# Attention inside a fused mixer: the second head's token halves on swapped partitions, score-value products in one lot

## The chip, the cores and the metric

The kernel runs on one core of one Trainium2 chip. The metric is the device time of one execution in microseconds (us). Before the change the median of three runs is 686.84 us (686.51 to 688.32).

## The reference, cut to what matters

```
# q, k, v, alpha: batch 4, heads 8, seq 768, head_dim 48
for t in range(S):
    state = alpha[:, :, t, :, None] * state + einsum('bhd,bhe->bhde', k[:, :, t], v[:, :, t])
    y[:, :, t] = einsum('bhd,bhde->bhe', q[:, :, t], state)
x = y with its heads side by side                      # 768 tokens x 384
u = x + (V^T U^T over the tokens) applied to x         # low rank, 32
x = u + relu(u @ w_ch1) @ w_ch2                        # hidden width 1536
theta = x @ w_theta;  y = w_tok_r (x cos theta) + w_tok_i (x sin theta)
u = x + y;  out = u + relu(u @ w_ch)
```

Everything is fp32. The large products are made from three products of split operands each (high x high, high x low, low x high).

## The kernel before, in words

**Units.** The attention of one batch element is worked off in eight units (`UNITS`): four pairs of heads, each in two halves of 384 tokens. A unit has three chunks (`c`) of 128 tokens, and each chunk has two sub-chunks of 64 tokens (`p` = 0, 1). The two heads of a pair are `h` = 0, 1. TensorE's array is used as four quarters of 64 x 64. A product's input partitions (0 to 63 or 64 to 127) choose the row of the quarter, its output partitions the column. All products of the attention are small, and each has two records in the profile, so a lot of 12 products shows as x24.

**The four steps of a unit on TensorE.**

- `pe_scores` (line 401): for each `h`, `p`, `c` it multiplies decayed keys (`k_end`) with an identity and the scaled queries (`ident_q`). This gives at once the keys turned round, so that tokens lie on partitions, and the scores. Input row `h`, output column `p`: all four quarters. Twelve products.
- `pe_state` (line 442): keys (`k_nat`) times values (`v_sb`), the contribution of each sub-chunk to the state. Input row `p`, output column `h`: all four quarters. Twelve products. It begins with a wait (below).
- the carried part of the output (line 491): scaled queries times the state before the sub-chunk. Row `h`, column `p`: four quarters. Twelve products for odd units; ten for even ones, whose first sub-chunk has no state before it.
- the score-value products (lines 497 and 507): masked scores (`probs`) times values. Row `p`, column `p`: only two of the quarters. Twelve products in two lots of six: line 497 in `pe_output_first`, line 507 in `pe_output_second`.

**Between them.** ScalarE copies the keys out of PSUM (`k_nat`, line 415), the state's contributions (`updates`, 463), the output (`x_nat`, 576). VectorE masks the scores (`probs`, 426) and runs three scans per unit (`tail` 342, `rel` 354, `state` 470). GpSimd makes `k_end` (379) and `ident_q` (370). SP issues all loads. `load_v` waits for `y_ready` of eight units earlier, and `queries` for an earlier `y_ready` as well.

**The first batch element** has nothing to hide behind. `pe_scores(u+1)`, some filling (two full-array products of `keep_warm`, line 1429, or part of the low-rank product, lines 589 and 643), `pe_output_first(u)` after `st_done`, `pe_state(u+1)`, a wait of TensorE for its own `half_done`, and `pe_output_second(u)` follow each other.

**The later three** are woven into the MLP of the element before. That MLP goes through 24 slots of 18 full-array products (lines 695 and 725). Every second slot ends with `pe_group(k)`, for `k` = 0 to 8, and group 9 comes in a slot near the end. Group `k` does the output of unit `k-2`, the scores of unit `k` and the state of unit `k-1`, as far as these exist. All operands are waited for ahead of the group (`group_ready`), so within a group TensorE waits only for its own earlier products. Those waits keep two row quarters from writing the same PSUM bank and partitions at once. Before the change they are: `half_done` (after line 497, ahead of `pe_state`) and `scores_ready` (ahead of line 507). Groups 2 to 7 have both, groups 8 and 9 only the first, groups 0 and 1 none.

**PSUM.** Later elements have banks 0, 1 and 2 for all of it. Scores of the two heads are in banks 0 and 2, the state's contributions of `p` = 0 and 1 in banks 0 and 1, the output of the two heads in banks 1 and 2. In every lot of the kernel before, products of row 0 and products of row 1 write different banks.

Of the kernel before, what the change touches and what calls it, by code (L numbers as in the profile page):

```python
# [61 lines left out]
def mixer_kernel(nc, qka, v_nat, u_w, v_w, w1, w2, w_theta, tok_r, tok_i, w_ch, out_t, x2_dram):  # L62
    ctx = ExitStack()
    with ctx:
# [210 lines left out]
        def y_ps(b, u):  # L275
            i, j = y_banks(b)
            return banks[:, i:j + 1, SCORES:SCORES + OUT].rearrange("p h (c n) -> p c h n", c=CPH)

        def updates_ps(b, u):
            (i, at), (j, to) = update_places(b, u)  # L280
            step = 512 * (j - i) + to - at
            two = banks[0:PAIR_ROWS, i:i + 2, :].rearrange("p i x -> p (i x)")
            if first_batch(b):
                two = two.rearrange("p (s x) -> p s x", s=2)[:, :, at:at + OUT]
            else:
                two = two[:, at:at + 2 * step].rearrange("p (s x) -> p s x", s=2)[:, :, 0:OUT]
            return two.rearrange("p s (c n) -> p n c s", c=CPH)
# [30 lines left out]
        def side(p):  # L318
            return slice(SUB * p, SUB * (p + 1))

# [69 lines left out]
        def pe_scores(pe, b, u):  # L390
            n, s = UNITS * b + u, u % 2
            i, j = score_banks(b, u)
            if first_batch(b):
                pe.wait_ge(S["k_end_done"], n + 1)
                pe.wait_ge(S["q_rel_done"], n + 1)
                wait(pe, S["updates_done"], updates_before(b, u - 1) if u else 0)
            for c in range(CPH):
                for p in range(2):
                    for h, ps in ((0, bank[i]), (1, bank[j])):
                        g = 2 * c + p  # L400
                        last = nc.tensor.matmul(ps[side(p), Q_STEP * c:Q_STEP * (c + 1)], k_end[s][rows(h), sub(g)],  # L401
                                                q_slot(u)[rows(h), g, :], stop=True, skip_group_check=True,
                                                start=first_batch(b) or c == 0 and (h == 0 or u < 2))
            return last
# [24 lines left out]

        def pe_state(pe, b, u):  # L430
            n, s = UNITS * b + u, u % 2
            if first_batch(b):
                pe.wait_ge(S["k_nat_done"], n + 1)
                pe.wait_ge(S["mask_done"], n + 1)
                pe.wait_ge(S[f"v_in{u}"], 16)
            for c in range(CPH):
                for p, (i, at) in enumerate(update_places(b, u)):
                    cols = slice(at + HEAD_DIM * c, at + HEAD_DIM * (c + 1))
                    for h in range(2):
                        at = HEAD_DIM * (CPH * h + c)  # L440
                        wide = HEAD_ROW if h == 0 else HEAD_DIM
                        last = nc.tensor.matmul(bank[i][HEAD_ROW * h:HEAD_ROW * h + wide, cols],  # L442
                                                k_nat[s][side(p), :, :, :].rearrange("p h c n -> p (h c n)")[:, at:at + wide],
                                                v_sb[u][side(p), c, HEAD_DIM * h:HEAD_DIM * (h + 1)],
                                                stop=True, skip_group_check=True,
                                                start=first_batch(b) or c == 0 and u == (0 if p else UNITS - 1))
            last.then_inc(S["ds_ready"], 1)
# [30 lines left out]
        def pe_output_first(pe, b, u):  # L478
            n, s = UNITS * b + u, u % 2
            y0, y1 = (bank[i] for i in y_banks(b))  # L480
            if first_batch(b):
                pe.wait_ge(S["st_done"], n + 1)
                wait(pe, S["y_done"], n)
            for c in range(CPH):
                for p in range(2):
                    g = 2 * c + p
                    if g == 0 and u % 2 == 0:
                        continue
                    begins = c == (1 if u % 2 == 0 and p == 0 else 0)
                    for h, ps in ((0, y0), (1, y1)):  # L490
                        nc.tensor.matmul(y_tile(ps, p, c), q_slot(u)[rows(h), g, HEAD_DIM:], state[s][rows(h), :, g + 1],  # L491
                                         start=begins, stop=False, skip_group_check=True)
            if first_batch(b):
                pe.wait_ge(S["mask_done"], n + 1)
            for c in range(CPH):
                for h, p, ps in ((0, 0, y0), (1, 1, y1)):
                    last = nc.tensor.matmul(y_tile(ps, p, c), probs[s][side(p), h, c, :],  # L497
                                            v_sb[u][side(p), c, HEAD_DIM * h:HEAD_DIM * (h + 1)],
                                            start=False, stop=True, skip_group_check=True)
            return last  # L500

        def pe_output_second(pe, b, u):
            s = u % 2
            y0, y1 = (bank[i] for i in y_banks(b))
            for c in range(CPH):
                for h, p, ps in ((0, 1, y0), (1, 0, y1)):
                    last = nc.tensor.matmul(y_tile(ps, p, c), probs[s][side(p), h, c, :],  # L507
                                            v_sb[u][side(p), c, HEAD_DIM * h:HEAD_DIM * (h + 1)],
                                            start=False, stop=True, skip_group_check=True)
# [28 lines left out]
        def pe_group(pe, b, k):  # L538
            n = UNITS * b + k
            if k > 1:  # L540
                pe_output_first(pe, b, k - 2).then_inc(S["half_done"], 1)
            if k < UNITS:
                pe_scores(pe, b, k).then_inc(S["scores_ready"], 1)
            if k > 1:
                pe.wait_ge(S["half_done"], n - 1)
            if 0 < k <= UNITS:
                pe_state(pe, b, k - 1)
            if 1 < k < UNITS:
                pe.wait_ge(S["scores_ready"], n + 1)
            if k > 1:  # L550
                pe_output_second(pe, b, k - 2)
# [880 lines left out]
        def _(pe):  # L1432
# [9 lines left out]
            for u in range(UNITS - 1):  # L1442
# [24 lines left out]
            pe_output_first(pe, 0, UNITS - 1).then_inc(S["half_done"], 1)  # L1467
            pe.wait_ge(S["x_t_done"], 1)
            lr_turn(pe, 0, 0, 2).then_inc(S["first_turned"], 1)
            pe.wait_ge(S["half_done"], UNITS)  # L1470
            pe_output_second(pe, 0, UNITS - 1)
# [57 lines left out]
```

## Time and profile before

| | |
|---|---|
| median of 3 runs | 686.84 us |
| profiled execution, own time | 687.91 us |
| its span from first to last instruction | 686.2 us |
| granted TensorE clock, mean | 0.993 |
| TensorE busy | 666.6 us (97%) |
| VectorE, ScalarE, GpSimd busy | 338.1, 246.5, 250.6 us |
| records of the attention's products | L401 768, L442 768, L491 704, L497 384, L507 384 |

"Busy" of TensorE counts overlapping products once, and it does not say whether one, two or four quarters work. For small products one has to look at the distance between the starts in the timeline.

### The profile page before, as it was taken

How to read it: one execution, taken by the hardware profiler on the slowest of the kernel's cores; microseconds unless marked ns; L12 is line 12 of the kernel's file. 1: busy time of each engine (PE TensorE's matmuls, PEld its weight loads, DVE VectorE, ACT ScalarE, POOL GpSimd, SP SyncE). 2: the span in 40 equal slices, each digit the busy share in tenths (PEclk: the TensorE clock that was granted, in tenths of full speed). 3: DMA queues.
4: the chain of work that ended last, by engine and by line, in shares of the span. 5: the costliest groups of instructions: out<-in, count | busy, mean ns of one | idle time of the engine just before them, and what ended most of it. 6: DMA issues, size and time to landing. Idle time of an engine off the chain costs nothing.

```text
span 686.2 us, 15688 instructions
## 1 busy us (share of the span) xinstructions
PE 666.6 (97%) x6360; PEld 639.2 (93%) x6360; DVE 338.1 (49%) x540; ACT 246.5 (36%) x519; POOL 250.6 (37%) x253
## 2 busy tenths in 40 slices
PE   7798999999999999999999999999999999999998
PEld 4477889999999999999999999999999999999998
DVE  7677786226555327555324124475545552554522
ACT  4464543323333223443223343435322431432220
POOL 5564763112333112333111364156332631643121
PEclk9899999999999999999999999999999999999999
DMA  9935613004414005401000643040022005002201
GB/s 254 238 105 129 182 42 115 1 2 126 108 39 115 1 2 146 111 15 37 1 1 35 230 128 93 1 149 24 1 81 104 23 11 172 23 0 69 70 0 70
DMA packets 25353, 52.36 MB, mean 76 GB/s; under 512 B 2144, under 2 KB 18128, under 8 KB 25296
## 3 DMA queue, kind: packets, MB, share of 16 engines
q1 hardware_dynamic: 25296, 51.52, 25.2%
q8 instruction: 45, 0.74, 0.5%
q14 instruction: 12, 0.10, 0.0%
HBM read 42.08 MB, written 9.44 MB: 75 GB/s over the span
## 4 chain that ended last, share of the span: by engine, by line
PE 89%; DVE 5%; issue 4%; ACT 2%; DMA 1%; SPq 0%; DVEq 0%; ACTq 0%
PE banks L695 21%; PE banks L1060 21%; PE banks L725 19%; PE banks L1132 6%; PE banks L978 5%; PE banks L491 3%; PE banks L401 3%; PE banks L1035 2%; PE banks L442 2%; PE banks L507 2%; PE banks L497 1%; PE banks L1429 1%; PE banks L643 1%; DMA qka_sb<-qka 1%; DVE rel L354 1%
## 5 line engine op out<-in xcount | busy, mean ns | idle before, releaser
L709 DVE SCALAR_TENSOR_TENSOR hidL<-banks,hidH 128x384 fp32r<-128x384 f32 x96 | 53.3, 555 | 119.9 <-ACT hidH L705 119.7
L695 PE MATMUL banks<-uH,w1H 128*128 128x384 f32 x288 | 100.0, 347 | 0.3 <-ACT uH L675 0.3
L725 PE MATMUL banks<-hidH,w2H 128*128 128x384 f32 x288 | 96.6, 335 | 1.3 <-ACT x_nat L576 0.7
L695 PE MATMUL banks<-uL,w1H 128*128 128x384 f32 x288 | 96.6, 335 | 0.0
L725 PE MATMUL banks<-hidH,w2L 128*128 128x384 f32 x288 | 96.5, 335 | 0.0
L695 PE MATMUL banks<-uH,w1L 128*128 128x384 f32 x288 | 96.5, 335 | 0.0
L725 PE MATMUL banks<-hidL,w2H 128*128 128x384 f32 x288 | 96.2, 334 | 0.0
L705 ACT ACTIVATE hidH<-banks 128x384 fp32r<-128x384 f32 x96 | 47.0, 490 | 117.9 <-PE banks L695 117.9
L379 POOL TENSOR_TENSOR k_end<-qka_sb,tail 112x384 f32<-112x384 f32 x32 | 30.0, 937 | 82.6 <-DVE tail L342 80.6
L1118 POOL TENSOR_TENSOR u2L<-x_res,u2H 128x384 fp32r<-128x384 f32 x24 | 24.4, 1017 | 95.5 <-ACT u2H L1112 95.5
L725 PEld LDWEIGHTS banks<-hidH,w2H 128*128 128x128 f32 x288 | 54.1, 188 | 2.7 <-issue 1.6
L695 PEld LDWEIGHTS banks<-uH,w1H 128*128 128x128 f32 x288 | 54.1, 188 | 2.5 <-issue 0.6
L695 PEld LDWEIGHTS banks<-uL,w1H 128*128 128x128 f32 x288 | 54.1, 188 | 0.3 <-DVE uL L680 0.3
L695 PEld LDWEIGHTS banks<-uH,w1L 128*128 128x128 f32 x288 | 54.1, 188 | 0.0
L725 PEld LDWEIGHTS banks<-hidL,w2H 128*128 128x128 f32 x288 | 54.1, 188 | 0.0
L725 PEld LDWEIGHTS banks<-hidH,w2L 128*128 128x128 f32 x288 | 54.1, 188 | 0.0
L354 DVE TENSOR_TENSOR_SCAN rel<-qka_sb,rel_start 112x390 f32<-112x390 f32 x32 | 52.9, 1653 | 1.4 <-DVE rel_start L350 0.3
L1060 PE MATMUL banks<-tokiH,ziH 128*128 128x384 f32 x144 | 49.4, 343 | 0.8 <-DVE tokiL L247 0.8
L1060 PE MATMUL banks<-tokrH,zrH 128*128 128x384 f32 x144 | 49.2, 342 | 0.0
L1060 PE MATMUL banks<-tokrH,zrL 128*128 128x384 f32 x144 | 48.4, 336 | 0.0
L1060 PE MATMUL banks<-tokrL,zrH 128*128 128x384 f32 x144 | 48.4, 336 | 0.0
L370 POOL TENSOR_TENSOR ident_q<-qka_sb,rel 112x384 f32<-112x384 f32 x31 | 30.1, 971 | 49.9 <-PE banks L507 26.7
(133 smaller groups left out, 1446.5 us busy)
## 6 DMA issues: line engine op xcount, KB each, us to landing
qka_sb<-qka SPq DMA_DIRECT2D x31, 507.1 KB, 6.4
v_sb<-v_nat SPq DMA_DIRECT2D x32, 144.0 KB, 6.5
stage<-w SPq DMA_DIRECT2D x6, 768.0 KB, 9.1
x_dram<-u_t SPq DMA_DIRECT2D x8, 576.0 KB, 3.7
x_f<-x_dram SPq DMA_DIRECT2D x12, 384.0 KB, 4.3
x_res<-x_dram SPq DMA_DIRECT2D x8, 576.0 KB, 4.3
out_t<-stage SPq DMA_DIRECT2D x24, 192.0 KB, 1.9
stage<-tok_r_t SPq DMA_DIRECT2D x3, 768.0 KB, 4.5
```

Source lines behind the costliest of these rows:

```text
L354: nc.vector.tensor_tensor_scan(flat(rel[0:PAIR_ROWS]), alpha_of(u)[:, 0:SCAN], rel_start[0:PAIR_ROWS, :], 0.0, ALU.mult, ALU.add).then_inc ...
L370: ops.tensor_tensor(q_slot(u)[0:PAIR_ROWS, :, HEAD_DIM:], q_of(u), rel[0:PAIR_ROWS, :, 1:SLOT], ALU.mult).then_inc(S["q_rel_done"], 1)
L379: nc.gpsimd.tensor_tensor(subs_of(k_end[s][0:PAIR_ROWS, :]), k_of(u), tail[s][0:PAIR_ROWS, :, 1:SLOT], ALU.mult).then_inc(S["k_end_done"], 1)
L401: last = nc.tensor.matmul(ps[side(p), Q_STEP * c:Q_STEP * (c + 1)], k_end[s][rows(h), sub(g)], q_slot(u)[rows(h), g, :], stop=True, skip_g ...
L695: last = nc.tensor.matmul(ps[:, 0:HALF], w[:, f, P * k:P * (k + 1)], x[half][:, k, :], start=(k == 0 and i == 0), stop=(k == DM_TILES - 1 ...
L705: nc.scalar.activation(hidH[s % 2][:], hid_ps[s % 2][:, 0:HALF], ACT.Relu).then_inc(S["hidH_done"], 1)
L709: nc.vector.scalar_tensor_tensor(hidL[s % 2][:], hid_ps[s % 2][:, 0:HALF], 0.0, hidH[s % 2][:].bitcast(F32), ALU.max, ALU.subtract).then_i ...
L725: last = nc.tensor.matmul(acc[m][:, 0:HALF], w[:, f, P * m:P * (m + 1)], x[s % 2][:], start=(f == 0 and i == 0), stop=(f == F_TILES - 1 an ...
L978: last = nc.tensor.matmul(th_ps[half][:, 0:HALF], w[:, k, P * m:P * (m + 1)], x[:, k, HALF * half:HALF * (half + 1)], start=(i == 0), stop ...
L1060: last = nc.tensor.matmul(tok_ps[half][:, 0:HALF], z[m][:, c, :], w[:, c, HALF * half:HALF * (half + 1)], start=(start and c == cs[0] and ...
L1118: nc.gpsimd.tensor_tensor(u2L[:, m, t], x_res[:, m, t], u2H[:, m, t].bitcast(F32), ALU.subtract).then_inc(S["u2L_done"], 1)
L1132: last = nc.tensor.matmul(ch_ps[t % 2][:, 0:HALF], w[:, k, P * m:P * (m + 1)], x[:, k, HALF * half:HALF * (half + 1)], start=(i == 0), sto ...
```

## The change

The second head of a pair keeps its two sub-chunks on swapped partitions. For `h` = 1 the scores, turned keys and values of sub-chunk `p` lie on the partitions of `1 - p` (`held(h, p)` = `side(p ^ h)`). The host lays `v_nat` out to match, at the same size. The score-value products then have input row `p ^ h` and output column `p`, and the state's contributions have input row `p ^ h` and output column `h`. The output and the state end where they did.

The score-value products become one lot of twelve (`pe_values`), which opens the output. The carried part (`pe_carried`) follows and ends it. A group's order is now: score-value products (unit `k-2`), state (unit `k-1`), carried part (unit `k-2`), scores (unit `k`). TensorE's waits for itself are `half_done` inside `pe_carried`, ahead of the first product with `(h, p)` = (1, 1), and `ds_ready` ahead of the scores. `half_done` is now given by one of the last four products of the state (by the last score-value product in group 9 and in the first element). Group 1 gets a wait it did not have. The banks of the later elements change places: scores in 1 and 2, output in 0 and 2, contributions in 0 and 1.

In the first element `pe_values` waits only for the mask and the output copy of the unit before. The wait for `st_done` stands in `pe_carried`.

```diff
         def score_banks(b, u):
-            return (i, i + 1) if first_batch(b) else (0, 2)
+            return (i, i + 1) if first_batch(b) else (1, 2)
         def update_places(b, u):
-            return ((i, SCORES), (i + 1, SCORES)) if first_batch(b) else ((0, SCORES), (1, 0))
+            return ((i, SCORES), (i + 1, SCORES)) if first_batch(b) else ((0, 0), (1, SCORES))
         def y_banks(b):
-            return (4, 5) if first_batch(b) else (1, 2)
+            return (4, 5) if first_batch(b) else (0, 2)
...
+        def held(h, p):
+            return side(p ^ h)
...
+        FOUR = ((1, 0), (0, 0), (1, 1), (0, 1))
+
         def pe_state(pe, b, u):
...
             for c in range(CPH):
-                for p, (i, at) in enumerate(update_places(b, u)):
+                for h, p in FOUR:
...
+                                            k_nat[s][held(h, p), :, :, :].rearrange("p h c n -> p (h c n)")[:, at:at + wide],
+                                            v_sb[u][held(h, p), c, HEAD_DIM * h:HEAD_DIM * (h + 1)],
...
+                    if not first_batch(b) and u and c == CPH - 1 and (h, p) == (1, 0):
+                        last.then_inc(S["half_done"], 1)
             last.then_inc(S["ds_ready"], 1)
...
+        def pe_values(pe, b, u):
+            n, s = UNITS * b + u, u % 2
+            if first_batch(b):
+                pe.wait_ge(S["mask_done"], n + 1)
+                wait(pe, S["y_done"], n)
+            for c in range(CPH):
+                for h, p in FOUR:
+                    last = nc.tensor.matmul(y_tile(bank[y_banks(b)[h]], p, c), probs[s][held(h, p), h, c, :],
+                                            v_sb[u][held(h, p), c, HEAD_DIM * h:HEAD_DIM * (h + 1)],
+                                            start=(c == 0), stop=False, skip_group_check=True)
+            return last
+
+        def pe_carried(pe, b, u):
+            n, s = UNITS * b + u, u % 2
+            if first_batch(b):
+                pe.wait_ge(S["st_done"], n + 1)
+            for c in range(CPH):
+                for h, p in FOUR:
+                    g = 2 * c + p
+                    if c == 0 and (h, p) == (1, 1):
+                        pe.wait_ge(S["half_done"], n + 1)
+                    if g == 0 and u % 2 == 0:
+                        continue
+                    last = nc.tensor.matmul(y_tile(bank[y_banks(b)[h]], p, c), q_slot(u)[rows(h), g, HEAD_DIM:],
+                                            state[s][rows(h), :, g + 1], start=False, stop=True,
+                                            skip_group_check=True)
             last.then_inc(S["y_ready"], 1)
...
         def pe_group(pe, b, k):
             n = UNITS * b + k
             if k > 1:
-                pe_output_first(pe, b, k - 2).then_inc(S["half_done"], 1)
-            if k < UNITS:
-                pe_scores(pe, b, k).then_inc(S["scores_ready"], 1)
-            if k > 1:
-                pe.wait_ge(S["half_done"], n - 1)
+                last = pe_values(pe, b, k - 2)
+                if k > UNITS:
+                    last.then_inc(S["half_done"], 1)
             if 0 < k <= UNITS:
                 pe_state(pe, b, k - 1)
-            if 1 < k < UNITS:
-                pe.wait_ge(S["scores_ready"], n + 1)
             if k > 1:
-                pe_output_second(pe, b, k - 2)
+                pe_carried(pe, b, k - 2)
+            if k < UNITS:
+                if k > 0:
+                    pe.wait_ge(S["ds_ready"], n)
+                pe_scores(pe, b, k).then_inc(S["scores_ready"], 1)
...
-                pe_output_first(pe, 0, u).then_inc(S["half_done"], 1)
+                pe_values(pe, 0, u).then_inc(S["half_done"], 1)
+                pe_carried(pe, 0, u)
                 pe_state(pe, 0, u + 1)
-                pe.wait_ge(S["half_done"], u + 1)
-                pe_output_second(pe, 0, u)
```

## Rows read from the trace of the kernel before

**Rows 1.** The page, its first line and the busy time of TensorE

```profile
span 686.2 us, 15688 instructions
PE 666.6 (97%) x6360; PEld 639.2 (93%) x6360; DVE 338.1 (49%) x540; ACT 246.5 (36%) x519; POOL 250.6 (37%) x253
```

**Rows 2.** Windows: length, busy of PE, PEld, DVE, ACT, POOL, clock, DMA, GB/s

```profile
0.00:54.00 54.00, 42.94 (x818) 31.12 (x819) 37.17 (x48) 27.60 (x62) 30.37 (x43) 0.91 0.75 201
54.00:82.00 28.00, 25.16 (x220) 22.63 (x220) 21.85 (x24) 13.00 (x31) 16.32 (x18) 1.00 0.52 140
...
88.00:190.00 102.00, 101.65 (x1224) 97.55 (x1225) 54.12 (x79) 36.33 (x85) 33.26 (x35) 1.00 0.24 70
```

**Rows 3.** Chain that ended last, 54 to 92 us: start, length, what

```profile
82.75 2.09 DVE rel L354
```

**Rows 4.** Groups by form: the two lots of score-value products

```profile
L497 PE MATMUL banks<-v_sb,probs 64*64 64x48 f32 x384 | 19.8, 221 | 0.0
L507 PE MATMUL banks<-v_sb,probs 64*64 64x48 f32 x384 | 18.1, 220 | 3.3 <-issue 3.1
```

**Rows 5.** Timeline of PE, group 1 of the second MLP: start, length, what

```profile
176.09 0.81 PE L401 MATMUL banks<-ident_q,k_end 48*64 48x112 f32 x24
176.71 0.50 PE L442 MATMUL banks<-v_sb,k_nat 64*64 64x48 f32 x24
177.15 0.45 PE L695 MATMUL banks<-uH,w1H 128*128 128x384 f32 x1
```

**Rows 6.** Timeline of PE, group 3, output of an odd unit

```profile
210.67 0.75 PE L491 MATMUL banks<-state,ident_q 48*64 48x48 f32 x24
211.23 0.46 PE L497 MATMUL banks<-v_sb,probs 64*64 64x48 f32 x9
...
212.10 0.56 PE L442 MATMUL banks<-v_sb,k_nat 64*48 64x48 f32 x23
212.47 0.55 PE L507 MATMUL banks<-v_sb,probs 64*64 64x48 f32 x12
212.95 0.44 PE L695 MATMUL banks<-uH,w1H 128*128 128x384 f32 x1
```

**Rows 7.** Timeline of PE, group 2, output of an even unit

```profile
202.02 0.65 PE L491 MATMUL banks<-state,ident_q 48*64 48x48 f32 x18
...
204.23 0.44 PE L695 MATMUL banks<-uH,w1H 128*128 128x384 f32 x1
```

**Rows 8.** Timeline of PE, group 8 (no scores)

```profile
236.83 0.65 PE L491 MATMUL banks<-state,ident_q 48*64 48x48 f32 x18
...
237.33 0.56 PE L497 MATMUL banks<-v_sb,probs 64*64 64x48 f32 x10
237.96 0.50 PE L442 MATMUL banks<-v_sb,k_nat 64*64 64x48 f32 x22
...
238.78 0.44 PE L695 MATMUL banks<-uH,w1H 128*128 128x384 f32 x1
```

**Rows 9.** Timeline of PE, group 9 (no scores, no state)

```profile
242.59 0.75 PE L491 MATMUL banks<-state,ident_q 48*64 48x48 f32 x24
243.14 0.54 PE L497 MATMUL banks<-v_sb,probs 64*64 64x48 f32 x12
243.73 0.55 PE L507 MATMUL banks<-v_sb,probs 64*64 64x48 f32 x12
244.22 0.44 PE L695 MATMUL banks<-uH,w1H 128*128 128x384 f32 x1
```

**Rows 10.** Chain that ended last, 0 to 60 us: a stall of TensorE

```profile
26.55 3.11 issue
```

**Rows 11.** Timeline of PE, last unit of the first element

```profile
50.21 0.75 PE L491 MATMUL banks<-state,ident_q 48*64 48x48 f32 x24 [0.39 <-DVE state L470]
50.77 0.53 PE L497 MATMUL banks<-v_sb,probs 64*64 64x48 f32 x12
...
51.70 0.55 PE L507 MATMUL banks<-v_sb,probs 64*64 64x48 f32 x12
```

More of the change, by code:

```diff
@@ L276, in y_ps @@
             i, j = y_banks(b)
-            return banks[:, i:j + 1, SCORES:SCORES + OUT].rearrange("p h (c n) -> p c h n", c=CPH)
+            return banks[:, i:j + 1:j - i, SCORES:SCORES + OUT].rearrange("p h (c n) -> p c h n", c=CPH)
         def updates_ps(b, u):
@@ L281, in updates_ps @@
             step = 512 * (j - i) + to - at
[L282 to L286, printed above, removed]
+            two = banks[0:PAIR_ROWS, i:i + 4, :].rearrange("p i x -> p (i x)")[:, 0:2 * step]
+            two = two.rearrange("p (s x) -> p s x", s=2)[:, :, at:at + OUT]
             return two.rearrange("p s (c n) -> p n c s", c=CPH)
@@ L400, in pe_scores @@
                         g = 2 * c + p
-                        last = nc.tensor.matmul(ps[side(p), Q_STEP * c:Q_STEP * (c + 1)], k_end[s][rows(h), sub(g)],
+                        last = nc.tensor.matmul(ps[held(h, p), Q_STEP * c:Q_STEP * (c + 1)], k_end[s][rows(h), sub(g)],
                                                 q_slot(u)[rows(h), g, :], stop=True, skip_group_check=True,
-                                                start=first_batch(b) or c == 0 and (h == 0 or u < 2))
+                                                start=first_batch(b) or c == 0 and u < 1 + h)
             return last
@@ L435, in pe_state @@
                 pe.wait_ge(S[f"v_in{u}"], 16)
+            places = update_places(b, u)
             for c in range(CPH):
-                for p, (i, at) in enumerate(update_places(b, u)):
+                for h, p in FOUR:
+                    i, at = places[p]
                     cols = slice(at + HEAD_DIM * c, at + HEAD_DIM * (c + 1))
[L439 to L446, printed above, removed]
+                    at = HEAD_DIM * (CPH * h + c)
+                    wide = HEAD_ROW if h == 0 else HEAD_DIM
+                    last = nc.tensor.matmul(bank[i][HEAD_ROW * h:HEAD_ROW * h + wide, cols],
+                                            k_nat[s][held(h, p), :, :, :].rearrange("p h c n -> p (h c n)")[:, at:at + wide],
+                                            v_sb[u][held(h, p), c, HEAD_DIM * h:HEAD_DIM * (h + 1)],
+                                            stop=True, skip_group_check=True,
+                                            start=first_batch(b) or c == 0 and (p == 1 or u == 0))
+                    if not first_batch(b) and u and c == CPH - 1 and (h, p) == (1, 0):
+                        last.then_inc(S["half_done"], 1)
             last.then_inc(S["ds_ready"], 1)
@@ L481, in pe_output_first @@
+        def pe_carried(pe, b, u):
+            n, s = UNITS * b + u, u % 2
             if first_batch(b):
                 pe.wait_ge(S["st_done"], n + 1)
-                wait(pe, S["y_done"], n)
             for c in range(CPH):
-                for p in range(2):
+                for h, p in FOUR:
                     g = 2 * c + p
+                    if c == 0 and (h, p) == (1, 1):
+                        pe.wait_ge(S["half_done"], n + 1)
                     if g == 0 and u % 2 == 0:
                         continue
[L489 to L509, printed above, removed]
+                    last = nc.tensor.matmul(y_tile(bank[y_banks(b)[h]], p, c), q_slot(u)[rows(h), g, HEAD_DIM:],
+                                            state[s][rows(h), :, g + 1], start=False, stop=True,
+                                            skip_group_check=True)
```

10 lines of the change are left out of this document (4 added, 6 removed).

## The prediction

> **What bounds the kernel now.** I read the page first: TensorE is busy for 666.6 of 686.2 us [rows 1]. Next I cut the span into stretches with their busy times [rows 2]. From 88 us on TensorE has hardly a gap (101.65 of 102.00 us), so every tenth of a microsecond taken from it there shortens the run. From 54 to 88 us it is different: TensorE has gaps, VectorE is busy for 21.85 of 28.00 us, and the chain of work runs through VectorE's scans until group 2 is past [rows 3]. Whatever TensorE gains or loses in groups 0, 1 and 2 of the first MLP is covered by them. Before 54 us TensorE, VectorE and the loads share the chain. Last I read the timeline of each kind of group. The three later elements repeat them to within 0.01 us, so one of each is shown [rows 5 to 9].
>
> **How a lot is priced.** A group costs from its first attention record to the next full-array record: 1.06 us for group 1 [rows 5], 2.28 for odd groups 3, 5, 7 [rows 6], 2.21 for even groups 2, 4, 6 [rows 7], 1.95 for group 8 [rows 8], 1.63 for group 9 [rows 9]. The pace of a lot is its length less the duration of one record, that is from first start to last start.
>
> - Six score-value products on two quarters (12 records) take 0.54 us with 0.22 for one record [rows 4, 9], a pace of 0.32. Twelve take 0.64 in two lots.
> - Twelve state products on four quarters (24 records of almost the same form) take 0.50 less 0.22 = 0.28 behind the scores [rows 5], and about 0.34 behind a wait or in a full group: 0.56 less 0.22 [rows 6], 0.50 less 0.22 for the first 22 of 24 [rows 8]. For twelve score-value products on four quarters I take 0.34, with 0.28 as the lower bound. The upper bound is the 0.64 of now.
> - The carried part has a pace of 0.48 (0.75 less 0.27), the scores 0.55 (0.81 less 0.26) [rows 5, 6].
> - A wait of TensorE for its own last product costs 0.28 from last start to next start: in group 9 the first lot ends at 243.68 and the next starts at 243.73, so 0.22 of record and 0.05 to 0.06 of waking [rows 9]. Without a wait a lot follows its predecessor in 0.02 to 0.07.
> - The full-array record behind a group starts 0.07 before the last small record ends: 242.59 to 244.22 against an end at 244.28 [rows 9].
>
> The Trainium skill ("TensorE: Matmul & The Clock Gate", section "Wait — 56ns, not 53.3ns?") says that starts never come closer than about 25 ns however small the product is. This trace disagrees: 24 starts in 0.28 us are 12 ns apart [rows 5]. By the page a lot of 24 would take an estimated 0.6 us, and four quarters would gain almost nothing; that is a rival below.
>
> **The change part by part.** The number of products, their shapes and all loads stay as they are. Work done by the host is no part of the time. ScalarE's copies read other banks with the same number of elements; I cost them at nothing, because ScalarE is busy for 36.33 of 102.00 us beside TensorE [rows 2], and if that cover were gone I would expect the same length of copy anyway.
>
> *Group 9.* Now: score-value 0.34, wait 0.28, carried 0.48, last record to full array 0.27 - 0.07 = 0.20. Sum 1.30 against 1.63: gain 0.33. (In an odd unit two carried products go ahead of the wait; that fills two quarters only, the other two still need their six records each, so I count nothing for it.)
>
> *Group 8.* Score-value 0.34, step 0.02, state 0.34, wait 0.26 (`half_done` comes from one of the last four state products, hardly earlier than the last one), carried 0.47, exit 0.20. Sum 1.63 against 1.95: gain 0.32. Before, this group had a bare wait too: the score-value lot ends at 237.89 and the state starts at 237.96 [rows 8].
>
> *Groups 2 to 7.* Before, both waits are hidden: other lots run between the product and the wait for it [rows 6]. Now the wait inside the carried part follows the state directly and is bare; the one for `ds_ready` ahead of the scores is hidden by the carried part. Score-value 0.34, step 0.02, state 0.34, wait 0.26, carried 0.47, step to the scores 0.08, scores 0.50 (no slow start behind a full-array product), exit 0.26 - 0.07 = 0.19. Sum 2.20 against 2.21 and 2.28: gain 0.01 in even and 0.07 in odd groups, 0.24 for the six. If the lots overlap better (state 0.28, wait 0.17) each gains 0.15 more; if each keeps a slow start, each loses 0.07.
>
> *Group 1.* State 0.34, a new bare wait 0.28, scores 0.55, exit 0.19. Sum 1.36 against 1.06: loss 0.30. Behind the waiting instruction stand only the scores, and ScalarE's and VectorE's work on them is due two slots later.
>
> *Three later elements.* 0.33 + 0.32 + 0.24 - 0.30 = 0.59 each, 1.8 in all. In the first MLP the loss of group 1 lies in the covered stretch: 0.3 back. So 2.1 us.
>
> *Order of the signals.* `scores_ready` still comes at the end of a group, where `y_ready` was; `y_ready` comes some 0.8 us earlier. ScalarE's first work after a group needs both, so it starts as before. `load_v` on SP and the queries on GpSimd wait for `y_ready` and can only go earlier. No queue is passed.
>
> *First element.* While TensorE is not waiting for `st_done` (units 0 to 4), the output costs 0.34 + 0.28 + 0.48 in place of 0.48 + 0.64 with its wait hidden: about even, at worst 0.1 us lost in each. Where it does wait for `st_done`, the score-value products now run ahead of that wait. In the last unit TensorE waits for VectorE's state [rows 11], and both lots behind it (0.32 each, with steps 0.8 in all) leave the chain, which from there runs through TensorE into the MLP. I take 0.8 - 0.3 = 0.5 us of gain, bounds -0.4 and +1.2. It passes through the covered stretch, since VectorE's chain there begins with the MLP.
>
> Sum: 2.1 + 0.5 = 2.6 us. The profiled execution's own time is 687.91 us (span 686.2), so it would be 685.3. The median of the runs is 1.07 us lower, 686.84, which gives **684.2 us**. With the bounds per group (+0.15 and -0.07, over nine groups in three elements +4 and -1.9, of which I believe half) this case alone spans 682.0 to 686.0.
>
> **The rivals.**
>
> - *The bare waits eat the gain (0.26).* The six middle groups are the weak term: 0.24 of gain rests on steps of 0.02 to 0.08. At 0.07 more in each of the 18, and nothing from the first element, 0.8 us are left: 686.0. For it: two hidden waits become one bare one, and group 1 gets a new one. Against it: groups 8 and 9 gain 0.3 each by rows alone.
> - *Two rows of quarters in one bank serialise (0.08), the case on the other side.* Before, products of row 0 and row 1 always write different banks within a lot. Now in the state and score-value lots both rows write into the same bank, in different partitions. No row shows that. If such products took turns, each lot of 24 would go at the two-quarter pace, 0.64 in place of 0.34: 0.3 us for eight state and eight score-value lots in each later element, 14.4 us, and some 2 us in the first, where only part of the lots lies on the chain: 686.84 - 2.6 + 16.4 = 700.6. It decides from 0.04 us a lot (2.6 us over 64 lots). The Trainium skill ("TensorEngine Tiling (Array Packing)", "Gotcha 1: PSUM Pressure") says that different row tiles cannot access the same PSUM bank at the same time, and does not say whether different partitions of it count. Nothing in this trace decides between them.
> - *A floor between starts (0.04).* If score-value products kept the pace of the scores (0.55) rather than the state's, 0.21 us for 24 units, 5.0 us, would be added: 689.2. Against it speaks the pace of the state [rows 5]. The 25 ns of the Trainium skill (the page and section above) would act in this way.
> - *Stalls of the first element move (0.10).* TensorE stands for 3.11 us in the middle of a lot, with no wait that a record names [rows 10], and its clock over the first 54 us is 0.91 [rows 2]. Such stalls may fall elsewhere with a new order of instructions, and a wait may then cover them or not: 3 us either way, 681.2 or 687.2, and in part with a lower clock behind them.
> - The likeliest case has 0.52.
>
> **How the numbers follow.** About 0.3%, 2.1 us, is what a measurement of this kernel can tell from no change. Of the likeliest case (centre 2.6 us of gain) most lies above it, but not all: 0.38 faster, 0.14 within. The waits' case: 0.05 faster, 0.17 within, 0.04 slower. Serialised and floor: slower, 0.12. Stalls: 0.06 faster, 0.02 within, 0.02 slower. Together faster 0.49, within 0.33, slower 0.18. The range is 681.4 to 687.6: it holds the first two cases and most of the stalls, and leaves out the 0.12 of the serialised cases.
>
> **What would show it.** In the profile after: groups 9 and 8 at 1.30 and 1.63, group 1 at 1.36, groups 2 to 7 all near 2.20 with no difference between odd and even; the score-value lot as x24 of some 0.56 us in length; a gap of 0.06 us between the state's end and the carried part. The state's pace tells of the bank: 0.34 as before, or 0.64. In the first element, full-array work should begin 0.5 us earlier than 53.5 us. The prediction is wrong if the six middle groups are off by more than 0.1 each, or if the first 54 us change by more than 1 us.

## The result, and the profile after

| | before | after |
|---|---|---|
| median | 688.32 us (5 runs, 686.51 to 689.11) | 682.64 us (5 runs, 681.54 to 684.83) |
| ratio | | 0.9938, 95% interval 0.9912 to 0.9964 |
| profiled execution, own time, span | 687.91, 686.2 | 684.83, 683.1 |

The change is faster by 0.6%, 4.3 us by the ratio and 5.7 by the medians. Two later sets with the same changed kernel gave 0.9917 (0.9896 to 0.9938) and 0.9931 (0.9906 to 0.9956). The kernel before had 56 runs in the three sets of experiments, with a median of 687.6 us. The changed kernel's medians were 682.14 and 683.46. So the gain is 4 to 6 us, where 2.6 was forecast; the interval of the first ratio alone reaches from 2.5 to 6.1 us. The profile of after is the slowest of its five runs, and it shows only 3.1 us of the gain.

The page of after, first line and busy times, against [rows 1]:

```profile
span 683.1 us, 15692 instructions
PE 663.4 (97%) x6360; PEld 631.3 (92%) x6360; DVE 337.3 (49%) x540; ACT 246.0 (36%) x519; POOL 250.3 (37%) x253
```

The timeline of TensorE in group 1 of the second MLP (start, length, what), against [rows 5], and below it the same group of the third:

```profile
175.05 0.56 PE L445 MATMUL banks<-v_sb,k_nat 64*48 64x48 f32 x24
175.69 0.81 PE L401 MATMUL banks<-ident_q,k_end 48*64 48x112 f32 x24
176.43 0.44 PE L694 MATMUL banks<-uH,w1H 128*128 128x384 f32 x1
...
275.61 0.56 PE L445 MATMUL banks<-v_sb,k_nat 64*48 64x48 f32 x24
```

The state ends at 175.61 and the scores begin at 175.69: this is the bare wait. The group takes 1.38 us where it took 1.06. From group 1 to group 1 of the next element it is 100.56 us. The kernel before starts the third MLP's group 1 at 277.66, 101.57 us after [rows 5]:

```profile
277.66 0.52 PE L401 MATMUL banks<-ident_q,k_end 48*64 48x112 f32 x12
```

So a later element is 1.01 us shorter. From the full-array product behind group 3 of the first MLP to the end of the span it is 592.2 us before and 589.0 after. The timeline of group 3 of after, against [rows 6]:

```profile
209.72 0.56 PE L490 MATMUL banks<-v_sb,probs 64*64 64x48 f32 x24
210.10 0.52 PE L445 MATMUL banks<-v_sb,k_nat 64*64 64x48 f32 x24
210.45 0.81 PE L506 MATMUL banks<-state,ident_q 48*64 48x48 f32 x22
...
211.12 0.81 PE L401 MATMUL banks<-ident_q,k_end 48*64 48x112 f32 x22
211.86 0.44 PE L694 MATMUL banks<-uH,w1H 128*128 128x384 f32 x1
```

The twelve score-value products are one lot of 24 records, 0.56 us long: a pace of 0.34 on four quarters. The state follows with 0.52 - 0.22 = 0.30, although rows 0 and 1 of the array now write into one bank. (In group 1, behind full-array products, it is 0.56 - 0.22 = 0.34.) The two carried products that are free of the wait start at 210.45. Group 2, 8 and 9 of after, the same view, against [rows 7], [rows 8] and [rows 9]:

```profile
201.12 0.57 PE L490 MATMUL banks<-v_sb,probs 64*64 64x48 f32 x24
201.51 0.52 PE L445 MATMUL banks<-v_sb,k_nat 64*64 64x48 f32 x24
202.01 0.66 PE L506 MATMUL banks<-state,ident_q 48*64 48x48 f32 x18
...
203.27 0.45 PE L694 MATMUL banks<-uH,w1H 128*128 128x384 f32 x1
...
235.47 0.56 PE L490 MATMUL banks<-v_sb,probs 64*64 64x48 f32 x24
...
237.03 0.45 PE L694 MATMUL banks<-uH,w1H 128*128 128x384 f32 x1
...
240.83 0.56 PE L490 MATMUL banks<-v_sb,probs 64*64 64x48 f32 x24
241.22 1.00 PE L506 MATMUL banks<-state,ident_q 48*64 48x48 f32 x24
242.15 0.44 PE L694 MATMUL banks<-uH,w1H 128*128 128x384 f32 x1
```

| group | before | forecast | after |
|---|---|---|---|
| 1 | 1.06 | 1.36 | 1.38 |
| 2, 4, 6 | 2.21 | 2.20 | 2.14 |
| 3, 5, 7 | 2.27 | 2.20 | 2.14 |
| 8 | 1.95 | 1.63 | 1.56 |
| 9 | 1.63 | 1.30 | 1.32 |

(Groups 3, 5 and 7 of before are 2.27 by the trace; the prediction's 2.28 is the difference of two rounded starts.) The gain is 0.21 in groups 2, 4 and 6, 0.40 in groups 3, 5 and 7, 0.39 in group 8 and 0.31 in group 9, less 0.32 in group 1: 1.0 us for each later element, in agreement with the period.

In the first element, the last unit's timeline, against [rows 11]:

```profile
49.90 0.56 PE L490 MATMUL banks<-v_sb,probs 64*64 64x48 f32 x24
50.57 0.76 PE L506 MATMUL banks<-state,ident_q 48*64 48x48 f32 x24
51.26 0.55 PE L642 MATMUL banks<-ident,x_nat 128*128 128x128 f32 x3
...
53.12 0.42 PE L694 MATMUL banks<-uH,w1H 128*128 128x384 f32 x1
```

The score-value lot lies ahead of the scan's end. From the carried part's start to the MLP's first product it is 2.55 us, where it was 53.5 - 50.21 = 3.3. The MLP begins only 0.4 us earlier than before, because the scan itself ends later (50.51 us against 50.16). Inside group 2 of the first MLP this execution has a stall, which the kernel before has not (chain of work, start, length, what):

```profile
83.10 1.35 issue
```

With it group 2 of the first MLP takes 3.89 us in place of 2.14.

### The profile page after: what moved, and what is told of

The parts are those of the page before. It is cut to its first block, busy times and chain, and to the rows that moved or that the text cites. A ratio compares the mean times of both kernels' runs of the same rounds, so it can differ in the third digit from the quotient of the medians.

```text
span 683.1 us, 15692 instructions
## 1 busy us (share of the span) xinstructions
PE 663.4 (97%) x6360; PEld 631.3 (92%) x6360; DVE 337.3 (49%) x540; ACT 246.0 (36%) x519; POOL 250.3 (37%) x253
## 4 chain that ended last, share of the span: by engine, by line
PE 93%; DVE 3%; issue 2%; ACT 1%; DMA 1%; SPq 0%; DVEq 0%; ACTq 0%
PE banks L694 23%; PE banks L724 21%; PE banks L1059 21%; PE banks L1131 6%; PE banks L977 5%; PE banks L506 3%; PE banks L401 3%; PE banks L1034 2%; PE banks L490 2%; PE banks L445 2%; PE banks L1428 1%; PE banks L642 1%; DMA qka_sb<-qka 1%; PE banks L588 1%; DVE tokiL L247 1%
## 5 line engine op out<-in xcount | busy, mean ns | idle before, releaser
L1059 PE MATMUL banks<-tokiL,ziH 128*128 128x384 f32 x144 | 48.3, 336 | 0.0
```

The source lines that it names most:

```text
L1059: last = nc.tensor.matmul(tok_ps[half][:, 0:HALF], z[m][:, c, :], w[:, c, HALF * half:HALF * (half + 1)], start=(start and c == cs[0] and ...
```

## The experiments

All times are medians. The kernel before is 687.85, 687.52 and 687.68 us in the three sets (e1 to e4, e5 to e8, e9 to e11).

### e1, e11: the changed kernel again

Edit: none.

> The changed kernel again, as the measure for the other three of this set. The theory (four quarters for the score-value lot, bare waits of TensorE for itself where hidden ones were) reads the changed kernel's groups from its own profile and expects them again to 0.01 us: 1.38 in group 1, 2.14 in groups 2 to 7, 1.56 in group 8, 1.32 in group 9, so 1.0 us gained in each later element. Whether the stall of 1.6 us between two starts inside group 2 of the first MLP, which the changed kernel's profile has and the kernel before has not, comes again is open: if it belongs to the new order it is there, if it is a matter of one execution it is not. Time expected 3 to 5 us under the kernel before.

> The changed kernel once more, beside these two. 4.5 to 6.5 us under the kernel before; no stall near 20 us; later elements as in its first profile to 0.02 us per group.

Measured: 682.14 us (6 runs, 679.75 to 684.41) and 683.46 us (8 runs, 680.73 to 685.66). e11 is 4.2 us under the kernel before, slightly less than expected. The groups repeat to 0.01 us, but for groups 2 and 3 of the first MLP. The stall in group 2 is absent from e1 and there again in e11, where the two groups take 3.07 and 2.50 us (chain of work, start, length, what):

```profile
81.82 0.53 issue
```

So it comes and goes with one and the same kernel. All profiles taken together, 7 of the 10 with the new order in the groups have it (after, e3, e4, e6, e7, e8, e11), e1, e2 and e10 have not, and none of the three with the old groups has it (the kernel before, e5, e9). The first product of the MLP comes at 50.59, 51.84 and, in the first profile, 53.12 us: the first element varies by 2.5 us with one kernel. From group 3 of the first MLP to the end the three profiles agree to 0.1 us.

### e2: the score-value lot head by head, on two quarters at a time

```diff
-            for c in range(CPH):
-                for h, p in FOUR:
+            for h in range(2):
+              for c in range(CPH):
+                for p in range(2):
                     last = nc.tensor.matmul(y_tile(bank[y_banks(b)[h]], p, c), probs[s][held(h, p), h, c, :],
```

> The same kernel, but the twelve score-value products are issued head by head: six of the first head on two quarters, then six of the second head on the other two. Products, waits and all other lots stay. Theory (the quarters are worth it): the lot takes the two-quarter pace, 0.64 in place of 0.35 us from first to last start, so each of groups 2 to 9 costs 0.2 to 0.3 more (the second half of the lot may run into the state's), 5 to 7 us over 24 units, and the whole change is lost: 1 to 3 us slower than the kernel before. Rival (the gain is in the order of the lots and one lot in place of two, not in the quarters): under 1 us of difference to the control.

Measured: 685.86 us, ratio to before 0.9972 (0.9955 to 0.9989), 3.7 us over the control. It was expected to be slower than the kernel before and is 2.0 us faster. Timeline of group 3 (start, length, what):

```profile
209.05 0.60 PE L491 MATMUL banks<-v_sb,probs 64*64 64x48 f32 x20
209.44 0.22 PE L445 MATMUL banks<-v_sb,k_nat 64*64 64x48 f32 x2
...
209.56 0.50 PE L445 MATMUL banks<-v_sb,k_nat 64*64 64x48 f32 x18
...
211.32 0.45 PE L695 MATMUL banks<-uH,w1H 128*128 128x384 f32 x1
```

The group takes 2.27 us, 0.13 more than with four quarters. The cost is half of what was expected, because the second head's six products run into the state's lot. With 0.12 to 0.13 for each of 24 groups that is 3.0 us: all that the later elements gain. From group 3 of the first MLP to the end it is 592.0 us, against 592.2 in the kernel before and 589.0 in the control. The quarters carry that gain, and the new order of lots alone gives nothing there. Yet the kernel stays 2 us under the one before. By this count the rest comes from the first element, which e9 tests.

### e3, e6: the old order in the first element alone

```diff
-                pe_values(pe, 0, u).then_inc(S["half_done"], 1)
-                pe_carried(pe, 0, u)
+                first_carried(pe, u)
                 pe_state(pe, 0, u + 1)
+                first_values(pe, u)
...
```

`first_carried` waits for `st_done` and gives `half_done`; `first_values` waits for `half_done` and gives `y_ready`. The last unit is changed in the same way.

> The changed kernel with the order of before in the first element alone: carried part after the state scan, the next unit's state, a wait for the carried part, then the twelve score-value products as one lot. The three later elements are untouched. Theory: in the last unit the score-value lot is back behind the scan and costs 0.4 to 0.6 us more from the scan's end to the MLP; units 0 to 4 are about even. So the first MLP product comes 0.3 to 0.6 us later than in the control and the time is 0.3 to 0.6 us longer. Rival (the order in the first element is worth nothing, loads and stalls decide there): the same start within 0.1 us.

> The kernel with the old order in the first element again, for a second profile. Theory: both stalls, the MLP begins between 53 and 56 us, against 50.5 to 53.1 us in the four profiles of the new order. Rival: no stall near 20 us, and a start within that band.

Measured: e3 685.46 us (7 runs, 683.26 to 689.18), ratio to before 0.9961 (0.9945 to 0.9978), 3.3 us over the control in the same set, where 0.3 to 0.6 was expected. e6, one execution: 686.76 us. The MLP begins at 56.05 in e3, whose profile is the slowest of its runs, and at 52.24 in e6; the latter lies under the expected band and inside that of the new order. Both profiles have a stall of TensorE near 20 us, 3.55 and 1.86 us long. Not all of the loss lies there: in both the stretch from the MLP's start through group 3 is longer too (table under e7).

### e5: the kernel before again

Edit: none.

> The kernel before, once more, for a second profile of its first 54 us. In its first profile TensorE stood twice with no wait that a record names: 1.7 us in the next unit's state products near 20 us and 3.1 us in the second score-value lot near 26 us. The profile of the kernel with the old order in the first element has both too (3.6 and 1.9 us); the four profiles with the new order have the second one alone. Theory (the early stall belongs to the old order): it is there again, 1.5 to 4 us long near 20 us, and the MLP begins between 52.5 and 56 us. Rival (chance): it is absent.

Measured: 685.98 us. The MLP begins at 51.58 us, 0.9 earlier than expected. The stall is there. It stands in TensorE's waits as "issue", in the middle of a lot of state products (timeline):

```profile
22.33 0.53 PE L442 MATMUL banks<-v_sb,k_nat 64*64 64x48 f32 x19 [1.82 <-issue]
```

### e7: only the wait moved, the new order of products kept

```diff
         def pe_values(pe, b, u):
             n, s = UNITS * b + u, u % 2
             if first_batch(b):
+                pe.wait_ge(S["st_done"], n + 1)
                 pe.wait_ge(S["mask_done"], n + 1)
```

> The changed kernel with the wait for the state scan moved ahead of the score-value lot in the first element; the order of the products is the new one. This splits the order from the wait. Theory A (the stall near 20 us comes when TensorE's instruction stream is held at the scan's wait ahead of the whole output, so that the next load of code is asked for late): the stall is back and the time is 2 to 3 us longer than the control's. Theory B (only the order of the products counts, or where the code is cut): no stall near 20 us; the time is 0.3 to 0.8 us longer, since the last unit's score-value lot (0.4) stands behind the scan again.

Measured: 685.88 us (12 runs), ratio to before 0.9980 (0.9957 to 1.0002). That is 3.7 and 2.4 us over the two controls, which ran in other sets, and 4.3 and 3.4 us by the ratios; 2 to 3 was expected. Of the two theories A is right as to the sign it named: the order of products is the new one, and the stall is back, at the same place in the stream of products (record 219 or 220 of TensorE's products in all five profiles that have it; timeline):

```profile
22.16 0.43 PE L507 MATMUL banks<-state,ident_q 48*64 48x48 f32 x9 [1.59 <-issue]
```

The DMA queues tell when the next piece of code was loaded. This is the view of the queues between 0 and 18.5 us, of e7 (its only line) and of the control e1:

```profile
q1 hardware_dynamic: 2041, 4.84, 92.6%
```

```profile
q1 hardware_dynamic: 2039, 4.82, 92.6%
q8 instruction: 1, 0.02, 0.3%
```

The loads in this time are the same to within two packets, and only the control has the instruction packet by then. All eight kernels with the score-value products ahead of the wait (the changed kernel and e1, e2, e4, e8, e9, e10, e11) have it before 18.5 us, and none of them stalls at this place of the stream. The five profiles with the wait ahead (the kernel before, e3, e5, e6, e7) have no such packet by 18.5 us and all stall there, for 1.6 to 3.6 us. The stall ends with the load: in these five traces the packet starts 2.6 to 3.0 us before the product at which TensorE stands. The same distance, 2.5 to 2.9 us, lies between the next packet and the end of the stall near 26 us, and between a later packet and the end of the stall in group 2 of the first MLP. Why the load is asked for later when TensorE is held ahead of the whole output is not shown by these runs.

That the wait's place costs time is shown by the medians. How much of it is the stall near 20 us is not. The profiles, cut at the MLP's first product and at the full-array product behind group 3 of the first MLP (us):

| | MLP begins | through group 3 | from there to the end |
|---|---|---|---|
| before, e5 | 53.49, 51.58 | 40.5, 40.5 | 592.2, 592.2 |
| e9 | 48.61 | 40.5 | 592.3 |
| after, e1, e11 | 53.12, 50.59, 51.84 | 41.0, 40.4, 40.7 | 589.0, 589.0, 588.9 |
| e3, e6 | 56.05, 52.24 | 42.2, 43.8 | 589.3, 589.0 |
| e7 | 51.83 | 42.3 | 589.1 |

e7 and the control e11 begin the MLP at the same time, although only e7 stood near 20 us. Of the 1.6 us between these two profiles 1.5 lie between the start of group 2 and the end of group 3 of the first MLP. There e7 has the stall of group 2 at twice the length, and behind it the granted clock is low, which it is not in e11 (chain of e7; windows of e7 and of e11 with length, busy of PE, PEld, DVE, ACT, POOL, clock, DMA, GB/s):

```profile
81.81 1.12 issue
```

```profile
83.00:86.40 3.40, 3.40 (x22) 3.25 (x22) 2.23 (x2) 0.96 (x4) 1.87 (x2) 0.64 0.02 6
```

```profile
82.40:86.00 3.60, 3.60 (x29) 3.42 (x29) 3.58 (x4) 2.06 (x6) 2.51 (x3) 1.00 0.01 5
```

e3 and e6 have such a low clock behind that stall as well (0.50 from 88 to 91 us, 0.59 from 85 to 89). In after, e11, e4 and e8, which have the stall too, the clock stays at 1.00 behind it. So what e3, e6 and e7 lose against the controls is in part a second loss, after the MLP's start. The kernel before does not have it, since its group 2 has no stall.

### e9: the new position in the first element, the old partitions

```diff
-                pe_output_first(pe, 0, u).then_inc(S["half_done"], 1)
+                first_values(pe, u)
+                first_carried(pe, u)
                 pe_state(pe, 0, u + 1)
-                pe.wait_ge(S["half_done"], u + 1)
-                pe_output_second(pe, 0, u)
...
```

`first_values` issues the twelve products on two quarters, ahead of the wait for the scan; `first_carried` waits for `st_done` and `half_done`. The last unit is changed in the same way.

> The kernel before, partitions and groups of the later elements as they were, but in the first element the twelve score-value products (on two quarters) go ahead of the wait for the state scan, and the carried part follows. Theory after the runs so far: about half of the change's gain is this position, not the swapped partitions, because TensorE no longer stands for 1.7 to 3.8 us near 20 us waiting for code. So the stall near 20 us is gone, the first packets of code beyond the preloaded ones come at 14 to 17 us rather than 19 to 22, and the time is 2.0 to 3.5 us under the kernel before. Rival: the stall's absence needs the new lot on four quarters or the other order of all lots; then the stall stays and the time is within 1 us of the kernel before.

Measured: 685.91 us (12 runs), ratio 0.9973 (0.9951 to 0.9994), 1.8 us under the kernel before (0.4 to 3.4 by the interval), a little less than expected. The stall near 20 us is gone, and the packet of code is there before 18.5 us. So the first element's part of the gain needs neither the swapped partitions nor four quarters. With the 3.0 us of the later elements it makes 4.8, against 4.2 to 5.7 of the controls. 1.8 us is also the length of the stall in the two profiles of the kernel before (1.67 and 1.82 us), but the gain is not that stall alone: the score-value products of the last unit leave the scan's path too, and a later wait can take up part of the stall. The chain of e9 shows what TensorE waits for next: the load of a unit's queries, keys and decays, then the scans (start, length, what):

```profile
7.24 11.76 DMA qka_sb<-qka
...
19.02 0.98 DVE tail L342
...
21.72 0.94 DVE state L470
```

### e4: the bare wait of groups 2 to 7 filled

```diff
...
+            score(b, k, 0, 1, 0)
+            for h, p, c in ((1, 0, first), (0, 0, first)):
+                carry(b, u, h, p, c)
+                todo.remove((h, p, c))
+            pe.wait_ge(S["vals_done"], (UNITS - 2) * (b - 1) + k - 1)
+            carry(b, u, 1, 1, 0)
+            todo.remove((1, 1, 0))
+            pe.wait_ge(S["half_done"], n - 1)
+            for x in todo:
+                last = carry(b, u, *x)
...
```

> The changed kernel with the bare wait of groups 2 to 7 filled: behind the state lot come one score product and up to three carried products that write no bank and partitions of the products waited for, one on each quarter; then the wait for half_done, the rest of the carried part and the rest of the scores. A second signal of TensorE to itself (after the score-value lot) covers the second head's carried product. Theory (the wait stands bare and costs its 0.2 us): groups 2 to 7 fall from 2.14 to 1.93 to 2.00 us, 18 of them, one of which lies under cover: 2.5 to 3.5 us under the control. Rival (a quarter is the bound, not the wait, or products are issued in order so that the fill pushes the rest back): groups stay at 2.10 or more and the time within 0.7 us of the control.

Measured: 680.10 us, ratio to before 0.9889 (0.9873 to 0.9906), 2.0 us under the control, where 2.5 to 3.5 was expected. Timeline of group 3 of the second MLP:

```profile
205.51 0.56 PE L522 MATMUL banks<-v_sb,probs 64*64 64x48 f32 x24
...
206.18 0.27 PE L408 MATMUL banks<-ident_q,k_end 48*64 48x112 f32 x1
206.19 0.26 PE L414 MATMUL banks<-state,ident_q 48*64 48x48 f32 x1
...
207.50 0.45 PE L731 MATMUL banks<-uH,w1H 128*128 128x384 f32 x1
```

The fill begins under the last state products (206.18), and the group takes 1.99 us in place of 2.14. Even groups take 1.96. Groups 2 and 3 of the first MLP did not gain: they take 3.35 and 2.31 us, with the stall that the changed kernel has there too. With 16 groups of 0.15 to 0.18 that is 2.6 us by the profile, and 2.0 by the medians. The wait stood bare, and 0.15 to 0.18 of its 0.21 us could be filled.

### e8, e10: less filling in the first element

```diff
-        KEEP_WARM = 2
+        KEEP_WARM = 1
```

(on the kernel of e4; 0 in e10)

> The kernel with the filled wait (680.1 us) and one filling full-array product in place of two in five units of the first element. Products that compute the result are all there. If TensorE bounds the first element, each product left out gives back 0.37 us (two records of 0.37 from start to start are one product of 0.75), 2 to 3.5 us in all. If VectorE's scans (4 us a unit) and the code loads bound it, nothing: within 0.7 us of 680.1. If the clock falls for lack of work, it is slower.

> The filled kernel with no filling full-array product at all in five units of the first element (two in the changed kernel, one in the run before this). One product less in each of five units gave 2.4 us. Theory (TensorE still bounds these units): 1 to 2.5 us more, 675.2 to 676.7. Rival (VectorE's scans take over, or the granted clock falls for lack of work): no gain or a loss against 677.7.

Measured: e8 677.67 us, ratio to before 0.9858 (0.9833 to 0.9884), the lowest median here. e10 681.90 us, 0.9907 (0.9875 to 0.9938), where 675.2 to 676.7 was expected. Windows (length, busy of PE, PEld, DVE, ACT, POOL, clock, DMA, GB/s) of e4, e8 and e10:

```profile
18.00:54.00 36.00, 31.34 (x655) 23.29 (x654) 22.99 (x32) 19.18 (x46) 20.04 (x19) 0.91 0.69 179
```

```profile
18.00:54.00 36.00, 31.59 (x641) 24.09 (x633) 24.74 (x35) 21.23 (x51) 21.57 (x21) 0.86 0.73 194
```

```profile
18.00:54.00 36.00, 28.63 (x612) 24.22 (x606) 20.18 (x30) 19.18 (x45) 21.82 (x20) 0.68 0.73 196
```

With one filling product left out of five units the time falls by 2.4 us by the medians and 2.1 by the ratios, whose intervals just overlap. That fits the theory that TensorE bounded these units, but does not show it. The five products, at 0.75 us each, make some 3.7 us of TensorE's time, the MLP begins 3.0 us earlier (47.50 against 50.49), and one of the stalls for code is 2.3 us shorter (timeline of e4, then of e8):

```profile
27.04 0.34 PE L477 MATMUL banks<-v_sb,k_nat 64*48 64x48 f32 x2 [2.61 <-issue]
```

```profile
25.22 1.39 PE L401 MATMUL banks<-ident_q,k_end 48*64 48x112 f32 x21 [0.34 <-issue]
```

With both left out more than the gain is lost. The granted clock is 0.68 of full speed over this stretch, and e10 also has two stalls that e8 has not (timeline):

```profile
33.05 0.55 PE L522 MATMUL banks<-v_sb,probs 64*64 64x48 f32 x9 [2.45 <-issue]
...
45.77 0.32 PE L477 MATMUL banks<-v_sb,k_nat 64*64 64x48 f32 x5 [1.47 <-issue]
```

Its MLP begins 3.9 us later than in e8, and the two stalls together are 3.9 us. How much the clock and how much the stalls cost is not separated by these runs.

## Why the prediction was right, and where it was not

- **Faster, by what was named.** The forecast was 684.2 us; measured were 682.64, and 682.14 and 683.46 later. The sign, the place (TensorE's groups in the later elements, the wait for the scan in the first) and the order of size held. The sum was too small by 1.7 us against the ratio's 4.3. Of this the later elements make 0.9 (2.1 was forecast; 3.0 us are gained there), and the first element the rest.
- **Groups 1, 8, 9.** Right to 0.02, 0.07 and 0.02 us. The new wait costs group 1 its 0.3 us.
- **Groups 2 to 7: mis-sized.** 0.24 us was forecast for the six, 0.61 measured. The state's pace is 0.30, not 0.34. The wait costs 0.20 to 0.21 from the state's last start to the carried part's first behind it, not 0.26: the product that gives `half_done` stands three before the last, and at 0.025 us from product to product three of them are the difference to the 0.28 of a wait for the last one. The other steps came out nearly as worked out: from the first score-value product to the state's first 0.39 (forecast 0.36), from the carried part's first product to the full-array one 1.26 (forecast 1.24).
- **First element: the step that failed.** In the last unit 0.7 us less lie between the scan and the MLP, where 0.8 was forecast. But "units 0 to 4 are about even" left out the stall near 20 us. The prediction had read only the one at 26.55 us [rows 10] and made moving stalls a rival of 0.10 in either direction. What happened is that rival's gaining side on top of the likeliest case: with the wait's new place the stall near 20 us is absent from every profile, with the old one (e7) it is back. By e9 the first element gains 1.8 us (0.4 to 3.4), not 0.5, which also is the prediction's own sign of being wrong (over 1 us in the first 54). Both misses, this one and the one in groups 2 to 7, go the same way, so they did not cancel. The stall near 26 us stays: it is 0.5 to 3.8 us long in the profiles with the new position and two units of filling, 1.9 to 3.1 with the old, and a change of it cannot be told from this spread.
- **The rival of the bare waits** was real as a cost: in e4, filling it gives 2.0 us. It did not eat the gain.
- **The rival of two rows in one bank** is ruled out here. The state lot went from 0.34 to 0.30 us in groups 2 to 8 although both rows of quarters write one bank, in different partitions. The page "TensorEngine Tiling (Array Packing)" of the Trainium skill ("Gotcha 1: PSUM Pressure") warns of the same bank at the same time. These runs show no cost while the partitions differ. Two rows on the same bank and partitions were not tried; the waits exclude it.
- **The floor between starts** is ruled out too: the score-value lot's 24 starts lie in 0.34 us, 15 ns apart. The 25 ns of the page "TensorE: Matmul & The Clock Gate" of the Trainium skill (section "Wait — 56ns, not 53.3ns?") do not hold for the products of this lot, which go to different quarters.
- **The cover from 54 to 88 us** was right in kind: from the MLP's start through group 3 the kernel before takes 40.5 us and e1 40.4, although e1 lost 0.32 in group 1. But the stretch also holds a loss that the prediction did not have: with the stall in group 2 it is 41.0 us in the profile of after and 40.7 in e11.

## What to carry to other kernels

When small products use only part of the array, look at which quarter each one takes: moving one operand to other partitions can fill the rest at no cost in products, here 0.12 to 0.13 us for each lot of twelve. A wait of TensorE for its own last products cost 0.2 to 0.3 us here where nothing else stood between the two. Put work there that conflicts with neither. And when an engine's queue must wait for another engine, put what does not need the result ahead of the wait. Here that was worth 1.8 us (0.4 to 3.4), and a stall for code went with it. Last, cut the profile into stretches before a gain is put down to one stall: e7 has the stall near 20 us and still begins the MLP when e11 does.

## What the runs showed of the hardware that was not expected

- TensorE's stall at a fixed place of its instruction stream (1.6 to 3.6 us) came in 5 of 5 profiles in which it was held ahead of the whole output in the first element, and in 0 of 8 in which some products stood ahead of the wait. In the eight, the first packet of the queue "instruction" came before 18.5 us. Three stalls of this kind end 2.5 to 3.0 us after such a packet's start, in every profile that has them.
- Behind the stall in group 2 of the first MLP the granted clock was 0.50 to 0.64 for some 3 to 4 us in e3, e6 and e7, and 1.00 in after, e4, e8 and e11, which have the stall too. Why is not shown.
- The same kernel begins its MLP between 50.59 and 53.12 us, takes 40.4 to 41.0 us from there through group 3, and is fixed to 0.01 us per group afterwards. So the spread of its three profiles is made in the first element and in groups 2 and 3 of the first MLP.
- Four quarters take products of 48 columns at 12 to 15 ns from start to start, while the same lot issued head by head costs only 0.13 us more, and records of the next lot start among its last ones.
